# The last tile of a mixture-of-experts kernel: half of its results made as rows, and a second engine that waits for the stores

## The reference

```python
def _moe2_ref(x, w_gate, w1, w2):            # x: 2304 x 512, 8 experts
    logits = x @ w_gate
    expert_idx = np.argmax(logits, axis=1)
    ...                                      # gate_w: softmax value of the chosen expert
    for e in range(E):
        mask = expert_idx == e
        ...
        xe = x[mask]
        h = np.maximum(xe @ w1[e], 0.0)      # 512 -> 1024
        ye = h @ w2[e]                       # 1024 -> 512
        out[mask] = gate_w[mask, None] * ye
    return out.astype(np.float32)
```

## Time and profile before

| | |
|---|---|
| median of 3 runs | 774.48 us (774.22 to 774.68) |
| the profiled execution's own time | 774.4 us |
| its span, first to last instruction | 772.6 us |
| mean granted clock of PE | 0.996 |
| PE busy | 756.1 us, 98% |
| DVE, ACT, POOL busy | 345.8, 315.4, 344.4 us |
| indirect transfers issued by GpSimd | 51 |

### The profile page before, as it was taken

The page is one execution under the profiler, slowest core; times in us unless marked ns, Lnnn a source line. Parts: engine busy times, 40 slices in busy tenths (PEclk is TensorE's granted clock), DMA queues, the critical chain, the costliest instruction groups (busy, mean ns, idle before and its releaser), DMA issues.

```text
span 772.6 us, 15056 instructions
## 1 busy us (share of the span) xinstructions
PE 756.1 (98%) x5328; PEld 675.7 (87%) x5329; DVE 345.8 (45%) x890; ACT 315.4 (41%) x688; POOL 344.4 (45%) x280
## 2 busy tenths in 40 slices
PE   7999999999999999999999999999999999999996
PEld 7988888888888888888888888998999999999996
DVE  6887878211124444244334446764962332332231
ACT  4888888333242222322242222454324325325220
POOL 6888992344223222222233222268727627538421
PEclk9999999999999999999999999999999999999998
DMA  8888771010040000200020000540172613521111
GB/s 333 299 278 292 276 279 53 28 54 28 1 190 28 1 1 0 109 0 0 0 83 28 1 1 0 187 172 29 31 260 98 204 55 122 163 61 31 31 61 33
DMA packets 26169, 75.30 MB, mean 97 GB/s; under 512 B 3200, under 2 KB 4096, under 8 KB 26000
## 3 DMA queue, kind: packets, MB, share of 16 engines
q1 hardware_dynamic: 22432, 64.13, 23.6%
q0 software_dynamic: 3264, 10.03, 4.3%
q10 hardware_dynamic: 432, 0.59, 0.2%
HBM read 61.11 MB, written 13.63 MB: 97 GB/s over the span
## 4 chain that ended last, share of the span: by engine, by line
PE 85%; DVE 5%; issue 3%; POOL 2%; ACT 2%; DMA 1%; POOLq 0%; DVEq 0%; SPq 0%; ACTq 0%
PE pj L755 25%; PE nm L967 13%; PE pj L1421 8%; PE nm L1465 6%; PE kv L967 6%; PE tr L967 6%; PE kv L1465 6%; PE nm L1421 5%; PE pj L269 2%; PE nm L347 2%; PE kv L285 1%; DVE pj L537 1%; PE pj L1478 1%; PE tr L1417 1%; DMA qk<-in_qk_n 1%
## 5 line engine op out<-in xcount | busy, mean ns | idle before, releaser
L940 POOL TENSOR_TENSOR gl<-sg,gh 128x512 fp32r<-128x512 f32 (+1 forms) x80 | 94.6, 1182 | 288.2 <-ACT gh L777 288.2
L771 DVE TENSOR_TENSOR sg<-pj,sg 128x512 f32<-128x512 f32 (+1 forms) x80 | 51.0, 637 | 212.8 <-ACT sg L764 212.6
L764 ACT ACTIVATE sg<-pj 128x512 f32<-128x512 f32 (+1 forms) x80 | 44.2, 553 | 143.4 <-PE pj L755 143.2
L755 PE MATMUL pj<-xh,win_h 128*128 128x512 f32 x256 | 100.0, 391 | 0.0
L755 PE MATMUL pj<-xh,win_l 128*128 128x512 f32 x256 | 99.6, 389 | 0.0
L755 PE MATMUL pj<-xl,win_h 128*128 128x512 f32 x256 | 99.6, 389 | 0.0
L777 ACT ACTIVATE gh<-sg 128x512 fp32r<-128x512 f32 (+1 forms) x80 | 47.2, 590 | 98.6 <-PE tr L967 61.1
L1421 PE MATMUL pj<-xTh,W 128*128 128x288 f32 x320 | 71.3, 300 | 0.2 <-DVE xTl L1694 0.2
L901 DVE SCALAR_TENSOR_TENSOR raw<-pj,xT 128x512 f32<-128x512 f32 x96 | 62.5, 689 | 19.7 <-ACT pj L842 13.2
L1225 POOL TENSOR_TENSOR W<-wraw,W 128x1024 fp32r<-128x1024 f32 x28 | 66.3, 2396 | 8.3 <-ACT W L1221 8.2
L755 PEld LDWEIGHTS pj<-xh,win_h 128*128 128x128 f32 x256 | 48.0, 188 | 10.0
(11 more groups left out here) (302 smaller groups left out, 1792.5 us busy)
## 6 DMA issues: line engine op xcount, KB each, us to landing
wraw<-in_moe_w SPq DMA_DIRECT2D x7, 2048.0 KB, 10.6
ve<-in_v_z SPq DMA_DIRECT2D x16, 585.0 KB, 4.4
qk<-in_qk_n SPq DMA_DIRECT2D x15, 576.0 KB, 6.3
qkT<-in_qk_t SPq DMA_DIRECT2D x15, 576.0 KB, 7.0
y_rows<-ys SPq DMA_DIRECT2D x18, 256.0 KB, 2.4
stage<-in_moe_w_in SPq DMA_DIRECT2D x8, 512.0 KB, 6.8
y_early<-ys SPq DMA_DIRECT2D x16, 256.0 KB, 2.9
stage<-in_moe_w_out SPq DMA_DIRECT2D x4, 512.0 KB, 6.0
```

Source lines behind the costliest of these rows:

```text
L755: mm = eng.matmul(ph[f % 3][:, 0:tiles_of(n) * P], w[f // F1A][:, c, f % F1A, :], x[:, c, :], start=(c == 0 and w is win_h and x is bh), s ...
L764: eng.activation(sg[f % 2][:, at], ph[f % 3][:, at], ACT.Sigmoid, scale=1.702).then_inc(a_sg, 1)
L771: eng.tensor_tensor(sg[f % 2][:, at], ph[f % 3][:, at], sg[f % 2][:, at], ALU.mult).then_inc(v_g, 1)
L940: eng.tensor_tensor(gl[f % 3][:, at], sg[f % 2][:, at], gh[f % 3][:, at].bitcast(F32), ALU.subtract).then_inc(g_gl, 1)
```

## The change

Two things are changed, and nothing ahead of the last tile's second product.

1. Chunks 2 and 3 of the last tile (features 256 to 511) are no longer made transposed. In `last_chunks` PE holds 96 tokens of hTh or hTl (a 128 x 96 block) and streams 256 columns of W2 past it, so that tokens lie on the partitions at once. This is done for each subtile in turn: 3 x 24 matmuls of 256 columns, into three free PSUM banks. Chunks 0 and 1 are made and turned as before; chunk 1 is turned in the middle of the first subtile's matmuls. ACT's copies and PE's turns of chunks 2 and 3 are gone. `result_last` now multiplies features 0 to 255 of all three subtiles, and then 256 to 511 of each as its matmuls end.
2. GpSimd waits for st_z to reach 48 behind its last transfer. SP still waits for it too.

```diff
--- before.py
+++ after.py
@@ -1073,8 +1073,8 @@
 
     MID, END = F2 // 2 - 1, F2 - 1
 
-    PARTS = (slice(0, (SUBS - 1) * SUB), slice((SUBS - 1) * SUB, TOK))
-    TURN = 2
+    LAST_D = DC // 2
+    CUT = LAST_D * P
 
     def sem(name):
         return ctx.enter_context(nc.semaphore(name))
@@ -1179,7 +1179,10 @@
     st_z = sem("st_z")
 
     def last_y(s, d):
-        return (ph[s][0:SUB, d * P:(d + 1) * P] if d < DC - 1 else (px, pr, pt)[s][0:SUB, 0:P])
+        return ph[s][0:SUB, d * P:(d + 1) * P]
+
+    def last_rows(s):
+        return (px, pr, pt)[s][0:SUB, 0:D - CUT]
 
     w1_v = w1.rearrange("e (c p) n -> e p c n", p=P)
     w2_v = w2.rearrange("e (f p) n -> e p f n", p=P)
@@ -1272,6 +1275,7 @@
                 eng.indirect_dma_start(out=out, out_offset=bass.IndirectOffsetOnAxis(ap=ocol_z[:, s:s + 1], axis=0),
                                        in_=ob[s][:, :], in_offset=None,
                                        bounds_check=bound[1], oob_is_err=False).then_inc(st_z, 16)
+            eng.wait_ge(st_z, 16 * SUBS)
 
         def ahead(eng, f):
             if f is None:
@@ -1478,36 +1482,26 @@
                 mm = eng.transpose(pt[0:SUB, d * P:(d + 1) * P], yTs[:, d, s * SUB:(s + 1) * SUB], ident[:, :])
             mm.then_inc(p_ty, 1)
 
-        def last_chunk(eng, t, k):
-
-
-
-            d = DC - 1
-            for part, at in enumerate(PARTS):
-
-                eng.wait_ge(a_yt, DC * t + d - 1 + part)
+        def last_chunks(eng, t, k):
+
+
+            eng.wait_ge(v_o, SUBS * t)
+            for s in range(SUBS):
                 for f in range(F2):
                     for w, h in ((HI, hTh), (HI, hTl), (LO, hTh)):
-                        mm = eng.matmul(py[(d + part) % 2][:, at], weights(w[1], f * D + d * P), h[:, f, at],
+                        mm = eng.matmul(last_rows(s), h[:, f, s * SUB:(s + 1) * SUB], W[:, w[1], f * D + CUT:(f + 1) * D],
                                         start=(f == 0 and w is HI and h is hTh), stop=(f == F2 - 1 and w is LO))
-                    if part == 0 and f == MID:
-                        turn_last(eng, t, d - 1)
-                    if part == 1 and f == TURN:
-                        turn_last(eng, t, d, range(SUBS - 1))
-                mm.then_inc(p_yy, 1)
-            turn_last(eng, t, d, range(SUBS - 1, SUBS))
-
-        def turn_last(eng, t, d, parts=range(SUBS)):
-
-
-            if d == DC - 1:
-                eng.wait_ge(v_o, SUBS * t)
-                eng.wait_ge(a_yt, DC * t + d + (1 if parts[0] == 0 else 2))
-            else:
-                eng.wait_ge(a_yt, DC * t + d + 1)
-            for s in parts:
+                    if s == 0 and f == MID:
+                        turn_last(eng, t, LAST_D - 1)
+                mm.then_inc(p_tz, 1)
+
+        def turn_last(eng, t, d):
+
+
+            eng.wait_ge(a_yt, DC * t + d + 1)
+            for s in range(SUBS):
                 mm = eng.transpose(last_y(s, d), yTs[:, d, s * SUB:(s + 1) * SUB], ident[:, :])
-                if d >= DC - 2:
+                if d == LAST_D - 1:
                     mm.then_inc(p_tz, 1)
 
         def ahead(eng, f):
@@ -1549,8 +1543,8 @@
             up(eng, 1, known[1], turns(1, True))
             def ending(t):
                 k = rank_of(eng, t)
-                down(eng, t, k, {(d + 1, MID): lambda d=d: turn_last(eng, t, d) for d in range(DC - 2)}, DC - 1)
-                last_chunk(eng, t, k)
+                down(eng, t, k, {(d + 1, MID): lambda d=d: turn_last(eng, t, d) for d in range(LAST_D - 1)}, LAST_D)
+                last_chunks(eng, t, k)
 
             last = known[0]
             with eng.Fori(2, FULL) as t:
@@ -1629,12 +1623,8 @@
             beside_tile(eng, 0, lambda k: highs(eng, k, 0, range(CHUNKS)))
             upper(1)
             tiles(eng, last, body)
-            for d in range(DC - 1):
+            for d in range(LAST_D):
                 leave(eng, last, d)
-
-            for part, at in enumerate(PARTS):
-                eng.wait_ge(p_yy, DC * last + DC + part)
-                eng.activation(yTs[:, DC - 1, at], py[(DC - 1 + part) % 2][:, at], ACT.Copy).then_inc(a_yt, 1)
 
         return ahead, late
 
@@ -1715,20 +1705,18 @@
         def result_last(eng, t):
 
 
-            cut = (DC - 1) * P
             link(eng, eng.tensor_copy(ocol_z[:, :], oid[:, bass.ds(SUBS * t, SUBS)]))
 
             eng.wait_ge(ld_x, 16 * SUBS * t + 2 * 16 * SUBS)
             for a in range(SUBS):
                 eng.wait_ge(st_o[a], 16 * t)
-            for part, first in ((slice(0, cut), 0), (slice(cut, D), SUBS)):
-                for s in range(SUBS):
-                    eng.wait_ge(p_tz, first + s + 1)
-                    done_y = last_y(s, DC - 1) if first else ph[s][0:SUB, part]
-                    ins = eng.tensor_scalar(ob[s][:, part], done_y, gates[:, bass.ds(SUBS * t + s, 1)], None,
-                                            ALU.mult)
-                    if first:
-                        ins.then_inc(v_z, 1)
+            eng.wait_ge(p_tz, SUBS)
+            for s in range(SUBS):
+                eng.tensor_scalar(ob[s][:, 0:CUT], ph[s][0:SUB, 0:CUT], gates[:, bass.ds(SUBS * t + s, 1)], None, ALU.mult)
+            for s in range(SUBS):
+                eng.wait_ge(p_tz, SUBS + s + 1)
+                eng.tensor_scalar(ob[s][:, CUT:D], last_rows(s), gates[:, bass.ds(SUBS * t + s, 1)], None, ALU.mult)\
+                   .then_inc(v_z, 1)
 
         def ahead(eng, f):
             if f is None:
```

## The result

The changed kernel takes 776.57 us (median of 12 runs, 775.5 to 778.0), the kernel before 774.74 in the same comparison (12 runs, 774.07 to 775.22): a ratio of 1.0020, 95% interval 1.0013 to 1.0028. That is 1.8 us slower where 1.1 was forecast, and just above the top of the range. Measured again in a later comparison it took 776.2 (8 runs) against 774.65: 1.0023 [1.0013, 1.0034], 1.55 us. The profiled execution took 777.07.

What follows compares the result with a forecast made beforehand. PE, busy 98% of the span, was taken to bound the kernel up to the end, where GpSimd's drain arrives last. First edit 0.9 us faster, second 2.0 to 2.1 slower: +1.1 on 774.48 gives 775.6 us, range 771.2 to 776.5.

Steps and rivals of the forecast that it cites:

- PE's pace: PE's new 256-column matmuls with 96 tokens held in the last tile: 120 ns each, within 112 to 133.
- DVE's last gating: DVE's final gating from PSUM, 256 columns: 475 ns, starting 0.32 us behind the start of PE's last instruction, at 764.62.
- The landing: Arrival of the last scatter's data: 2.8 us after the scatter's start at 765.94, so at 768.74 against 769.7 before.
- Wait to drain: At the block's end, GpSimd needs 0.16 us from the landing to its drain's start, as SP did: 768.90.
- Drain to the span's end: Release of the block's end barrier after GpSimd's drain: 0.55 us.
- The drain: GpSimd's drain at the block's end: 4.24 us of its own work, now behind the landing, 768.90 to 773.14; chance 0.46.
- rival A: GpSimd's end drain is short once all has landed, 0.19 to 0.5 us: 771.5 us in total; chance 0.28.
- Rival B: GpSimd's end drain waits for an event 2.3 us behind the landing: 773.5 us; chance 0.15 together with Rival D.
- Rival C: GpSimd's end drain does 5.40 us of work from its own start, now behind the landing: 776.8 us; chance 0.11.
- Rival D: GpSimd's added wait changes nothing, only the first edit's 0.9 us gain counts: 773.5 us; chance 0.15 together with Rival B.
- PE's arrival: PE reaching the block's end moves with its last matmul, from 769.4 to about 768.4, ahead of GpSimd's.
- The sum: Whole tail: first edit gives 0.9 us, second takes 2.0 to 2.1, together +1.1; span 773.7 against 772.6.

## Why the prediction was right or wrong

The mechanism was the forecast one, and none of the rivals; the loss came out at 1.8 us, and 1.55 when measured again, instead of 1.1, at the bound of 1.55 between "same" and "slower". (Of the 0.97 between 775.6 and 776.57, 0.26 is the kernel before, which took 774.74 in this comparison.) The forecast gave this mechanism a chance of 0.46. Its 83 ns for each transfer rested on one drain, which work, a late event and polling all fitted; only the experiments made it more than a guess that came true. Step by step, by the prediction's own terms:

- PE's pace. Forecast 120 ns within 112 to 133; it was 118. The chunk's last matmul starts 8.69 us behind its first, forecast 764.30 - 755.45 = 8.85. Right, and 0.16 on the good side. No slower weight load showed with 96 tokens held, as the sum had it.
- DVE's last gating: 0.48, forecast 0.475. To the scatter's start 0.83, forecast 0.84. From the chunk's start the scatter comes 10.32 behind, forecast 10.49, before 11.40: the first edit brought it forward by 1.08, not 0.91, of which the products are 0.49 and the copy and turn that went 0.59.
- The landing: forecast 2.8, and it was 3.06 (767.30 to SP's branch at 770.4). This is the one term in the touched stretch that was mis-sized. I took it for a lone transfer's; on the same stretch PE's jump fetches code through one of the same DMA engines. That this lengthens a landing rests on the one kernel without the jump (2.75, against 3.0 to 3.3 in the eight with it); how much of the 0.26 here is the fetch is not shown.
- Wait to drain: 0.14 instead of 0.16. Drain to the span's end: 0.56 instead of 0.55.
- The drain: forecast 4.24 as work, measured 4.236. The reason given, 51 transfers of 83 ns each, also held: 48, 42 and 3 transfers since the last drain took 4.07, 3.64 and 0.29 to 0.40. The Trainium skill (PSUM — Partial Sum Buffer, Engine vs sequencer instructions) has a drain wait for the engine to go idle; here GpSimd had been idle for over 2 us and its drain still took 4.2, so the measurement decides, and rival A falls. Rival B falls with the wait alone, where the drain went on 4.2 us behind the landing, not 2.3. Rival C would have shown 5.4. Rival D falls because GpSimd's drain began behind the landing, at 770.5.
- PE's arrival, forecast at 768.4, some 4 us behind its last matmul, came 1.5 behind it (765.67 to 767.2): with no wait for ACT left, its sequencer was in the jump 2 us before that matmul began. It cost nothing, as it was not the last to arrive.
- The sum of these, 1.2 in the touched stretch, against 1.1 forecast: 0.16 too much for PE and 0.26 too little for the landing nearly cancel, and this closeness is luck.

What the sum left out is the rest of the program: I took everything ahead of 755.45 to stay as it was in time. In the profiled execution it was 1.5 us late. By medians, the wait alone costs 2.7 where its stretch shows 2.0, and the two edits 1.8 and 1.55 where theirs shows 1.2. These excesses of 0.4 to 0.7 us are within the noise: the 95% intervals reach down to 1.2 us for the wait alone and to 1.0 for the two edits.

How late a profiled execution came was settled far ahead of the change. At the `feat` turns the traces of the changed kernel and of the wait alone stood 1.5 and 1.7 late (56.30 and 56.57), that of the early drain 0.3 (55.19), that of no drain 0.5 (55.31), and the changed kernel measured again was 0.25 early (54.60). The two late ones were late for different reasons, a load in the one and the lower clock level from 12 us on in the other. No trace joins either to the edit, and the changed kernel's second trace has neither. Whether the kernels with the wait meet such delays more often cannot be told from one profile for each; the mean clocks of the wait alone hint at it. They are 0.992 to 0.995 in its twelve executions, 0.995 to 0.997 for the changed kernel; the four at 0.995 took 776.4 to 777.2 us, the three at 0.992 and 0.993 took 777.6 to 778.8. But a longer end in which PE idles lowers the mean too, so this stays open.

## What to carry to other kernels

Ask of a wait at a block's end what its engine has still to do behind it: GpSimd's drain took some 0.08 us for each transfer that it had issued since its last one, and this is partly hidden while the last transfer is in flight. So put no wait ahead of it; better still, put a drain into an earlier gap of GpSimd, where it costs nothing, and the last one shrinks to the landing; this was worth 2.5 us to the kernel before and 4.7 to the changed one. If such a tail is worth a few tenths per cent, measure each edit of a pair alone: here a gain of 1.0 was hidden by a loss of 2.7.

## What the runs showed of the hardware

- GpSimd's drain costs about 0.08 us for each indirect transfer issued since the last drain: 4.24 for 51, 4.07 for 48, 3.64 for 42, 0.29 to 0.40 for 3. With few of them it ends 0.15 us behind their landing. At the block's end no other engine's drain was above 0.52 us, but for PE's 2.3 in the kernel without the jump, where it waited for PE's last matmuls.
- A jump of PE over a long branch took 3.4 us at the end of the changed kernel, and a 16 KB fetch of code went with it. A 96-row scatter beside it landed in 3.0 to 3.3 us, without jump and fetch in 2.75, and in 4.4 beside two fetches; the kernel before landed in 2.85 beside one.
- From 12 to 16 us in one trace (the wait alone) PE's granted clock was 0.52 to 0.63, the lower of its two levels for most of that time, behind a wait of 1.72 us; it cost 1.6 us.
- An fp32r matmul with 96 tokens held and 256 columns starts every 118 ns, against 120 with 128 held and 112 in bf16.
